# First channel product of a one-core attention and mixer kernel in seven block products, with pieces of the second between them

## The chip, the cores and the metric

The kernel runs on one core of one Trainium2 chip, in fp32 from end to end as the caller sees it. The metric is the device time of one execution in microseconds, the median of three runs. The engines are TensorE (PE, with its weight loads PEld), VectorE (DVE), ScalarE (ACT), GpSimd (POOL) and the DMA queue of SyncE (SP).

## The reference, cut to what matters

Three stages follow each other: a windowed attention, a mixer with a token and a channel part, and a gated channel block. The change lies in the channel part of the mixer (`_moe_ref`). The input `x` is the attention's output, 2 batches x 768 tokens x 512.

```python
def _moe_ref(x, w_tok1, w_tok2, w_ch1, w_ch2):
    xt = x.transpose(0, 2, 1)
    h = np.maximum(xt @ w_tok1, 0.0) @ w_tok2
    u = x + h.transpose(0, 2, 1)
    h2 = np.maximum(u @ w_ch1, 0.0) @ w_ch2      # 512 -> 1536 -> 512
    return u + h2

def _moe2_ref(x, mu_k, mu_r, w_k, w_v, w_r):
    ...
    k = np.maximum(xk @ w_k, 0.0)
    v = k * k @ w_v
    r = 1.0 / (1.0 + np.exp(-(xr @ w_r)))
    return r * v
```

## The kernel before

Every product runs on PE in fp32r. To keep precision each operand is split in a high half (rounded to fp32r) and a low half (the rest), and `three` (L944 to L948) issues high x high, high x low and low x high into the same PSUM bank. Making the halves is elementwise work: a copy that rounds (ACT, DVE or POOL) and a subtraction (DVE or POOL).

Tokens are cut in four groups g of 384 (`GR`), two to a batch; `u` holds, by 128 channels kk (`KT` = 4), the transposed activations. The order of work on each engine is written by hand, engine by engine, with semaphores between them; there is no scheduler. The stages that matter:

- Token stage (about 98 to 131 us): for 16 tiles, PE transposes x (L1017), multiplies the token part, DVE adds into `u` (L812). Beside it the weights of the channel part are split: DVE rounds (L794), POOL subtracts (L484). Between tiles 4 and 5 stand 36 matmuls of 512 columns of the token part's first product.
- Channel stage, L1034 to L1069: a loop over g. For each of 12 tiles f of 128 hidden channels, `first(f)` multiplies 4 kk x 3 matmuls of 384 columns into bank f % 2, ACT makes `rH` = ReLU (L614), DVE `rL` (L845), and `second(f - 1)` adds 4 x 3 matmuls of 384 columns into banks 2 to 5. All of W1 and half of W2 stand in SBUF with both halves before the stage begins; POOL makes the rest (L482, L484) early in it.
- Last stage, from about 332 us: a loop over g with `hidden(f)`, 12 matmuls of 384, and `value(f)`, 9 of 512, and the gate's 36 of 512. DVE has `k` (L871), `k2L` (L874), and the mixing of tokens (L833, L839).

Of the kernel before, what the change touches and what calls it, by code (L numbers as in the profile page):

```python
# [18 lines left out]
def build_program(nc, q, k, v, w_tok1, w_tok2, w_ch1, w_ch2, mu_k, mu_r, w_k, w_v, w_r, out):  # L19
# [28 lines left out]
    UG = GR + 1  # L48
    WIDE = 1024
    NWT, N1, N2, NK, NR, NV = 6, FC // 2, FC // 2, FK // 2, KT // 2, FK // 2  # L50

    ctx = ExitStack()
    with ctx:
# [32 lines left out]
        AS = 2 * N1 * W + 2 * 3 * W  # L86
        U0 = A0 + AS
        US = 4 * KT * NGR * UG
# [43 lines left out]

        reg = Region(A0, AS)
        W1H = reg.take("W1H", [P, N1, WIDE], F32R)
        W1L = reg.take("W1L", [P, N1, WIDE], F32R)
        W2aH = reg.take("W2aH", [P, 3, WIDE], F32R)
        W2aL = reg.take("W2aL", [P, 3, WIDE], F32R)
        reg = Region(X0, XS)
        W2bH = reg.take("W2bH", [P, 3, WIDE], F32R)
        W2bL = reg.take("W2bL", [P, 3, WIDE], F32R)  # L140
        WkH = reg.take("WkH", [P, NK, WIDE], F32R)
        WrH = reg.take("WrH", [P, NR, WIDE], F32R)
        reg = Region(T0, TS)
        uH = reg.take("uH", [P, KT, GR], F32R)
        uL = reg.take("uL", [P, KT, GR], F32R)
        WrL = Region(T0 + TS // 2, TS // 2).take("WrL", [P, NR, WIDE], F32R)
        WkL = Region(H0, HS).take("WkL", [P, NK, WIDE], F32R)

        reg = Region(A0, AS)
        xkH = reg.take("xkH", [P, KT, GR], F32R)  # L150
# [3 lines left out]
        assert reg.pos <= A0 + 5 * W  # L154
# [3 lines left out]
        k2 = [reg.take(f"k2{i}", [P, GR]) for i in range(2)]  # L158
        k2H = [reg.take(f"k2H{i}", [P, GR], F32R) for i in range(3)]
        k2L = [reg.take(f"k2L{i}", [P, GR], F32R) for i in range(3)]  # L160
        assert reg.pos <= A0 + 2 * N1 * W

        reg = Region(X0 + W, 2 * W)
        sg = [reg.take(f"sg{i}", [P, DM]) for i in range(RT)]
        u = at("u", [P, KT, NGR, UG], U0)
        reg = Region(H0, HS)
        h1H = reg.take("h1H", [P, B, TT, DM], F32R)
        h1L = reg.take("h1L", [P, B, TT, DM], F32R)
        reg = Region(R0, RS)
# [29 lines left out]
        wh_done, wp_done, wl_done = sem("wh_done"), sem("wp_done"), sem("wl_done")  # L199
# [81 lines left out]
        def w_dst(n):

            if n < PC2:
                return W1H[:, n - PC1, :], W1L[:, n - PC1, :]
            if n < PK:
                j = n - PC2
            elif n < PR:
                return WkH[:, n - PK, :], WkL[:, n - PK, :]
            elif n < PV:
                return WrH[:, n - PR, :], WrL[:, n - PR, :]  # L290
            else:
                j = n - PV
            return (W2aH[:, j, :], W2aL[:, j, :]) if j < 3 else (W2bH[:, j - 3, :], W2bL[:, j - 3, :])
# [3 lines left out]
        def _(sp):  # L297
# [62 lines left out]
            def load_piece(n, slot, src, by_rows, j, free=True):  # L360
                if free:
                    sp.wait_ge(wl_done, n - NSTG + 2)
                if by_rows:
                    dst, part = halves(stg[slot][:, :]), src[:, bass.ds(2 * j, 2), :]
                else:
                    dst, part = quarters(stg[slot][:, :]), src[:, :, bass.ds(256 * j, 256)]
                sp.dma_start(dst, part).then_inc(ld_w[slot], 16)

            sp.wait_ge(wl_done, NWT + 1)
            for slot in range(NSTG):  # L370
                load_piece(PC1 + slot, slot, w1_cols, False, slot, free=False)
            for slot in range(NSTG):
                load_piece(PC1 + NSTG + slot, slot, w1_cols, False, NSTG + slot)
            with sp.Fori(0, N2 // NSTG) as i:
                for slot in range(NSTG):
                    load_piece(PC2 + NSTG * i + slot, slot, w2_rows, True, NSTG * i + slot)
            for n in range(PK, PEND):
                first, src, by_rows = ((PK, wk_cols, False) if n < PR else (PR, wr_rows, True) if n < PV
                                       else (PV, wv_rows, True))
                load_piece(n, (n - PC1) % NSTG, src, by_rows, n - first)  # L380
# [10 lines left out]
        def _(pool):  # L391
# [96 lines left out]
        def _(act):  # L488
# [35 lines left out]
            for credited in (xl_done, av_done, wl_done, vs_summed, wr_done, o_done, x2_done, sg_done, mixl_done):  # L524
                act.sem_inc(credited, 1)
# [619 lines left out]
```

## Time and profile before

| what | us |
|---|---|
| runs, device time | 505.86, 504.46, 503.38; median 504.46 |
| span of the profiled execution | 501.4 |
| PE busy | 478.4 (95%) |
| DVE, ACT, POOL busy | 221.7, 191.6, 114.6 |
| channel stage, 131.4 to 331.9 | 200.5, of which PE busy 200.5 |

The profile is of one execution. Its own device time is not given beside its span; the median of the runs is 3.0 us above the span. Times within the trace count from the span's start. A matmul's end is modelled, so "busy" on PE does not say how fast it works; the distance between two starts does. A line number such as L948 is that of a helper where one issues many matmuls.

### The profile page before, as it was taken

Reading aid. Unit: us, or ns where it says so; the run is one execution under the profiler, and the core shown is the slowest. Engines: PE = TensorE matmul, PEld = TensorE weight load, DVE = VectorE, ACT = ScalarE, POOL = GpSimd, SP = SyncE. Lnnn points to the kernel's source line nnn. Section 1 sums busy time; section 2 is a strip of 40 time slices with the busy share of each in tenths; the row PEclk is TensorE's granted clock in tenths of the full one; section 3 lists DMA queues with packets and bytes.
Section 4 is the critical chain, followed back from the end, with each engine's and each line's share of the span. In section 5 each row is a group of like instructions: output and inputs, shape, how many; then the busy total and the mean of one; then the engine's idle time right before and its main releaser. Section 6 shows DMA issues by size and latency. Waiting matters only on the chain.

```text
span 501.4 us, 8399 instructions
## 1 busy us (share of the span) xinstructions
PE 478.4 (95%) x2968; PEld 444.9 (89%) x2968; DVE 221.7 (44%) x575; ACT 191.6 (38%) x424; POOL 114.6 (23%) x98
## 2 busy tenths in 40 slices
PE   4798789998999999999999999999999999999996
PEld 4677678787999999999999999999889989989985
DVE  5598887499411141114111411456436355444521
ACT  3799887424211121112111211345455256353411
POOL 6364553285999000000000024300000000000000
PEclk9999999999999999999999999999999999999999
DMA  9999997144443100000000010000010001001001
GB/s 196 181 208 215 228 213 186 46 126 129 166 149 145 43 1 0 0 0 0 0 0 0 0 42 0 0 1 0 1 49 14 0 21 42 0 0 63 0 0 63
DMA packets 48657, 31.70 MB, mean 63 GB/s; under 512 B 21248, under 2 KB 42496, under 8 KB 48640
## 3 DMA queue, kind: packets, MB, share of 16 engines
q1 hardware_dynamic: 48640, 31.49, 26.4%
q8 instruction: 9, 0.15, 0.1%
q14 instruction: 8, 0.07, 0.1%
HBM read 27.14 MB, written 3.15 MB: 60 GB/s over the span
## 4 chain that ended last, share of the span: by engine, by line
PE 84%; SPq 5%; DMA 5%; ACT 2%; issue 2%; DVE 1%; POOL 0%; ACTq 0%; POOLq 0%
PE bank L946 26%; PE bank L947 26%; PE bank L948 26%; DMA kn<-in_k_dram 4%; SPq L301 2%; PE bank L998 1%; SPq L310 1%; DMA v<-in_v_dram 1%; PE bank L976 1%; ACT e_sb L518 1%; PE bank L1017 1%; ACT qbd L498 1%; PE bank L895 1%; SPq L321 1%; PE bank L928 1%
## 5 line engine op out<-in xcount | busy, mean ns | idle before, releaser
L845 DVE SCALAR_TENSOR_TENSOR rL<-bank,rH 128x384 fp32r<-128x384 f32 x48 | 26.7, 557 | 148.2 <-ACT rH L614 148.2
L614 ACT ACTIVATE rH<-bank 128x384 fp32r<-128x384 f32 x48 | 23.6, 492 | 163.1 <-PE bank L948 158.7
L946 PE MATMUL bank<-uH,W1H 128*128 128x384 f32 x192 | 64.8, 337 | 0.0
L947 PE MATMUL bank<-uL,W1H 128*128 128x384 f32 x192 | 64.6, 336 | 0.0
L948 PE MATMUL bank<-uH,W1L 128*128 128x384 f32 x192 | 64.4, 336 | 0.0
L947 PE MATMUL bank<-xkL,WkH 128*128 128x384 f32 x128 | 43.3, 338 | 0.0
L946 PE MATMUL bank<-xkH,WkH 128*128 128x384 f32 x128 | 43.1, 337 | 0.0
L948 PE MATMUL bank<-xkH,WkL 128*128 128x384 f32 x128 | 42.8, 335 | 0.0
L947 PEld LDWEIGHTS bank<-uL,W1H 128*128 128x128 f32 x192 | 36.1, 188 | 0.0
L948 PEld LDWEIGHTS bank<-uH,W1L 128*128 128x128 f32 x192 | 36.0, 188 | 0.0
L946 PEld LDWEIGHTS bank<-uH,W1H 128*128 128x128 f32 x192 | 36.0, 188 | 0.0
L482 POOL CAST W2aH<-stg 128x1024 fp32r<-128x1024 f32 x3 | 3.1, 1040 | 142.3 <-PE bank L948 142.3
L871 DVE SCALAR_TENSOR_TENSOR k<-bank,kr 128x384 f32<-128x384 f32 x32 | 17.8, 556 | 38.7 <-ACT kr L631 38.6
L948 PE MATMUL bank<-rH,W2aL 128*128 128x384 f32 x96 | 32.3, 336 | 0.0
L948 PE MATMUL bank<-rH,W2bL 128*128 128x384 f32 x96 | 32.3, 336 | 0.0
L946 PE MATMUL bank<-rH,W2bH 128*128 128x384 f32 x96 | 32.2, 335 | 0.0
L947 PE MATMUL bank<-rL,W2bH 128*128 128x384 f32 x96 | 32.2, 335 | 0.0
L946 PE MATMUL bank<-rH,W2aH 128*128 128x384 f32 x96 | 32.2, 335 | 0.0
L947 PE MATMUL bank<-rL,W2aH 128*128 128x384 f32 x96 | 32.2, 335 | 0.0
L631 ACT ACTIVATE kr<-bank 128x384 f32<-128x384 f32 x32 | 15.7, 489 | 43.1 <-PE bank L948 42.7
L518 ACT ACTIVATE e_sb<-s_sb,nmx 128x120 f32<-128x120 f32 x96 | 29.7, 382 | 3.3 <-DVE nmx L693 3.3
L928 PE MATMUL bank<-kw,qbd 128*128 128x120 f32 x192 | 27.6, 292 | 1.8 <-ACT qbd L498 1.6
(131 smaller groups left out, 1093.2 us busy)
## 6 DMA issues: line engine op xcount, KB each, us to landing
stg<-in_moe_w_ch_dram SPq DMA_DIRECT2D x12, 512.0 KB, 3.6
vw<-in_v_dram SPq DMA_DIRECT2D x16, 240.0 KB, 4.9
kn<-in_k_dram SPq DMA_DIRECT2D x16, 192.0 KB, 3.8
qn<-in_q_dram SPq DMA_DIRECT2D x16, 192.0 KB, 4.4
v<-in_v_dram SPq DMA_DIRECT2D x16, 192.0 KB, 5.1
out_dram<-o_sb SPq DMA_DIRECT2D x12, 256.0 KB, 2.0
stg<-in_moe_w_k_dram SPq DMA_DIRECT2D x4, 512.0 KB, 3.5
stg<-in_moe_w_v_dram SPq DMA_DIRECT2D x4, 512.0 KB, 3.4
```

Of the source, the lines that this page charges most:

```text
L301: sp.dma_start(dst[par][:, h, :, :], src[bass.ds(2 * p + h, 1)].rearrange("o p t n -> (o p) t n")).then_inc(loaded[par], 16)
L310: sp.dma_start(dst, src[bass.ds(2 * p + h, 1)].rearrange("o p t n -> (o p) t n")).then_inc(ld_vw[par], 16)
L321: sp.dma_start(vw[par][LOC:COLS, :, :, :].rearrange("p t h n -> p t (h n)"), vsb[par][:, :, :].rearrange("p h n -> p (h n)").unsqueeze(1) ...
L518: act.activation(e_sb[par][:, n, :], s_sb[r][:, n, :], ACT.Exp, bias=nmx[:, r, n:n + 1], scale=-1.0).then_inc(exp_done, 1)
L614: act.activation(rH[f % 2][:, :], bank[f % 2][:, 0:GR], ACT.Relu).then_inc(rh_done, 1)
L631: act.activation(kr[f % 2][:, :], bank[f % 2][:, 0:GR], ACT.Relu).then_inc(kr_done, 1)
L845: dve.scalar_tensor_tensor(out=rL[f % 2][:, :], in0=bank[f % 2][:, 0:GR], scalar=0.0, in1=rH[f % 2][:, :].bitcast(F32), op0=ALU.max, op1=A ...
L871: dve.scalar_tensor_tensor(out=k2[f % 2][:, :], in0=bank[f % 2][:, 0:GR], scalar=0.0, in1=kr[f % 2][:, :], op0=ALU.max, op1=ALU.mult).then ...
L928: ins = pe.matmul(bS[gp][:, COLS * n:COLS * n + COLS], qbd[par][:, t, :], kw[par][:, t, :], start=True, stop=True)
L946: pe.matmul(dst, wH, mH, start=start, stop=False, **more)
L947: pe.matmul(dst, wH, mL, start=False, stop=False, **more)
L948: return pe.matmul(dst, wL, mH, start=False, stop=stop, **more)
```

## The change

The first channel product is computed by Strassen's scheme (in the form with shared sums) on 2 x 2 blocks. A block of W1 is 256 channels by 128 hidden channels, a block of u 256 channels by 384 tokens, so one run of the scheme (a "quad" q, 12 in all, 6 for each batch) makes two tiles of hidden channels for a whole batch of 768 tokens. Seven block products, each 2 x 3 matmuls of 384 columns, take the place of eight. `PRODUCTS` gives, for each, which sum of W1, which of u, the bank, and whether it opens or closes an accumulation.

- The seven combinations of W1 for a quad are made during the quad before: POOL does four sums of 256 columns (`sums_w1`), ACT rounds (`high_w1`), DVE subtracts (`low_w1`: 512, 256 and 1024 columns). W1 is read from HBM once for each batch, so there are 12 pieces in place of 6. The seven of u are made once for each batch: POOL `combine_u` (768 columns, 4 of them), ACT `high_u`, DVE `low_u`; batch 0's in the token stage, batch 1's in quads 0 to 5.
- Banks 0 and 1 hold sums that are shared, so products wait for DVE and ACT to have read a bank in the middle of a quad. DVE makes u2, u3, c22, c21 and c12 from a bank and an SBUF tile; ACT and DVE make the high and low half of R11 from the bank and of R22, R21, R12 from SBUF.
- The second product of quad q - 1 is cut in eight chunks, each 3 x (512 + 256) columns for one of two f and one of four d, which stand between the products of quad q as `GAPS` says; in the first quad of batch 1 as `GAPS_LAST` says.
- W2 is split anew for each batch by POOL (12 pieces); the weights of the last stage, which were split early in the channel stage, now come after it or between (`SLOT2`, `TAIL`): three in quads 6 to 8, seven behind the last product.
- DVE's residual adds are 512 and 2 x 256 columns wide and, for batch 0, stand in quad 6.

```diff
-            def channel(g):
-                def first(f):
...
-                    for kk in range(KT):
...
-                        ins = three(bank[f % 2][:, 0:GR], W1H[:, f // 2, c:c + P], W1L[:, f // 2, c:c + P],
-                                    uH[:, kk, :], uL[:, kk, :], kk == 0, kk == KT - 1)
...
+            def product(q, n):
+
+                b, slot = q // NFP, q % 2
+                w, m, bk, start, stop = PRODUCTS[n]
+                if n == 0:
+                    pe.wait_ge(w1_split, q + 1)
+                    if q:
+                        pe.wait_ge(sum_done, 5 * q)
+                if q % NFP == 0:
+                    pe.wait_ge(ul_done, NPROD * b + U_PLACE[m] + 1)
+                if n + 1 == P2:
+                    pe.wait_ge(p1_done, q + 1)
+                elif n + 1 == P7:
+                    pe.wait_ge(sum_done, 5 * q + 1)
+                elif n + 1 == P5:
+                    pe.wait_ge(rl_done, 4 * q + R11)
+                elif n + 1 == P4:
+                    pe.wait_ge(sum_done, 5 * q + 2)
+                elif n + 1 == P3:
+                    pe.wait_ge(sum_done, 5 * q + 3)
+                for kk in range(2):
+                    ins = three(bank[bk][:, 0:GR], w1H[slot][:, w, kk, :], w1L[slot][:, w, kk, :],
+                                ucH[b][:, m, kk, :], ucL[b][:, m, kk, :], start and kk == 0, stop and kk == 1,
+                                skip_group_check=True)
+                ins.then_inc(prod_done, 1)
...
+            GAPS, GAPS_LAST = (1, 1, 1, 1, 1, 1, 2), (2, 2, 2, 1, 1, 0, 0)
+            for q in range(NQ):
+                todo = list(CHUNKS) if q else []
+                for n in range(NPROD):
+                    product(q, n)
+                    for _ in range((GAPS_LAST if q == NFP else GAPS)[n] if q else 0):
+                        second(q - 1, *todo.pop(0))
+            for f, d in CHUNKS:
+                second(NQ - 1, f, d)
...
+            def quad(q):
...
+                plus(P6, u2, Bk, p1)
+                low_r(R11, 0, 0, A)
+                plus(P7, u3, Bk, p1)
+                if 1 <= q < NQ - 1:
+                    low_w1(q + 1, 0)
+                if q == NFP:
+                    residual(0, 0)
...
+                plus(P5, c22, A, u3)
+                low_r(R22, 1, 1, c22[:, :])
+                if q == NFP:
+                    residual(0, 1)
+                plus(P4, c21, Bk, p1)
+                if 1 <= q < NQ - 1:
+                    low_w1(q + 1, 1)
+                low_r(R21, 1, 0, c21[:, :])
+                for i in ahead:
+                    low_u(1, i)
+                if q == NFP:
+                    residual(0, 2)
+                plus(P3, c12, A, u2)
+                low_r(R12, 0, 1, c12[:, :])
+                if q == NFP:
+                    residual(0, 3)
```

The order of products is P1, P6, P2, P7, P5, P4, P3; P1, P2, P5 and P3 go to bank 0, P6, P7 and P4 to bank 1. The products' names and the sums' stand for their place in the scheme.

DVE in the channel stage before, two tiles of it (`rL` is the low half of the ReLU; the number behind a name tells buffers apart). This pattern fills a group:

```order
L845 SCALAR_TENSOR_TENSOR rL_130<-bank,rH_128 128x384
L844 REGISTER_ALU
L845 SCALAR_TENSOR_TENSOR rL_131<-bank,rH_129 128x384
L844 REGISTER_ALU
L845 SCALAR_TENSOR_TENSOR rL_130<-bank,rH_128 128x384
```

DVE now, from P6 to P3 of quad 2 (`u_111` is u2, `u_112` u3, `p_110` P1's copy, `c_113` c22, `c_101` c21, `c_105` c12, `ucL` the low half of batch 1's blocks):

```order
L1007 TENSOR_TENSOR u_111<-bank,p_110 128x384
L1012 SCALAR_TENSOR_TENSOR rL_108<-bank,rH_106 128x384
L1007 TENSOR_TENSOR u_112<-bank,p_110 128x384
L941 TENSOR_TENSOR w1L_97<-stg_56,w1H_93 128x512
L944 TENSOR_TENSOR w1L_97<-stg_56,w1H_93 128x256
L1007 TENSOR_TENSOR c_113<-bank,u_112 128x384
L1012 SCALAR_TENSOR_TENSOR rL_108<-c_113,rH_106 128x384
L1007 TENSOR_TENSOR c_101<-bank,p_110 128x384
L947 TENSOR_TENSOR w1L_97<-w1S_96,w1H_93 128x1024
L1012 SCALAR_TENSOR_TENSOR rL_108<-c_101,rH_106 128x384
L955 TENSOR_TENSOR ucL_104<-u,ucH_102 128x768
L1007 TENSOR_TENSOR c_105<-bank,u_111 128x384
```

One instruction of a tile has become a row of twelve (with the low half of R12 behind them thirteen), in which two inputs of most rows lie in SBUF.

POOL in the channel stage before (`stg` holds a weight as it came from HBM):

```order
L482 CAST W2bH<-stg_55 128x1024
L484 TENSOR_TENSOR W2bL<-stg_55,W2bH 128x1024
L482 CAST W2bH<-stg_56 128x1024
L484 TENSOR_TENSOR W2bL<-stg_56,W2bH 128x1024
L482 CAST W2bH<-stg_57 128x1024
L484 TENSOR_TENSOR W2bL<-stg_57,W2bH 128x1024
L482 CAST WkH<-stg_55 128x1024
L484 TENSOR_TENSOR WkL<-stg_55,WkH 128x1024
```

POOL now, from quad 2 on (`w1S` are sums of W1, `ucT` those of u, `w2` the piece of W2):

```order
L543 TENSOR_TENSOR w1S_96<-stg_56 128x256
L544 TENSOR_TENSOR w1S_96<-stg_56 128x256
L546 TENSOR_TENSOR w1S_96<-w1S_96,stg_56 128x256
L548 TENSOR_TENSOR w1S_96<-stg_56,w1S_96 128x256
L570 CAST w2H_117<-stg_57 128x1024
L572 TENSOR_TENSOR w2L_119<-stg_57,w2H_117 128x1024
L563 TENSOR_TENSOR ucT_103<-u,ucT_103 128x768
```

What was one run of splits at the stage's start is spread over all quads, with the sums ahead of each.

PE, a product of quad 1 and the piece behind it, where before 12 matmuls of `W1H` and 12 of `W2` followed each other:

```order
L1131 MATMUL bank<-ucH_98,w1H_93 128x384
L1132 MATMUL bank<-ucL_100,w1H_93 128x384
L1133 MATMUL bank<-ucH_98,w1L_97 128x384
L1264 MATMUL bank<-rH_106,w2H_117 128x512
L1265 MATMUL bank<-rH_106,w2H_117 128x256
L1264 MATMUL bank<-rL_108,w2H_117 128x512
L1265 MATMUL bank<-rL_108,w2H_117 128x256
L1264 MATMUL bank<-rH_106,w2L_119 128x512
L1265 MATMUL bank<-rH_106,w2L_119 128x256
```

Half of the second product's matmuls are now 512 columns wide, half 256, each pair with the same weights.

## Rows read from the trace of the kernel before

**Rows 1.** the page: the span and the chain that ended last:

```profile
span 501.4 us, 8399 instructions
...
PE 84%; SPq 5%; DMA 5%; ACT 2%; issue 2%; DVE 1%; POOL 0%; ACTq 0%; POOLq 0%
```

**Rows 2.** busy us (count) by stretch; then PE's clock, DMA share, GB/s:

```profile
98.00:131.40 33.40, 31.02 (x185) 28.38 (x181) 30.34 (x35) 10.62 (x22) 24.16 (x11) 1.00 0.41 127
131.40:331.90 200.50, 200.50 (x1154) 200.50 (x1153) 45.69 (x83) 33.56 (x69) 43.64 (x26) 1.00 0.09 29
331.90:373.30 41.40, 41.40 (x206) 37.08 (x205) 20.86 (x38) 18.32 (x35) 0.00 (x0) 1.00 0.02 9
```

**Rows 3.** PE in order of time: start, duration; 36 matmuls' first, and their follower:

```profile
103.63 0.39 PE L946 MATMUL bank<-xH,wt1H 128*128 128x512 f32 x1
...
111.83 0.49 PE L1017 MATMUL bank<-ident,u 128*128 128x128 f32 x3
```

**Rows 4.** weight loads: groups (busy us, mean ns), and eight by time:

```profile
L947 PEld LDWEIGHTS bank<-uL,W1H 128*128 128x128 f32 x192 | 36.1, 188 | 0.0
...
L928 PEld LDWEIGHTS bank<-kw,qbd 128*128 128x128 f32 x192 | 25.6, 208 | 2.4 <-issue 2.0 <-DVE nmx L693 0.4
...
27.20 0.97 PEld L928 LDWEIGHTS bank<-kw,qbd 128*128 128x128 f32 x8
```

**Rows 5.** groups of DVE and ACT by shape: busy us, mean ns:

```profile
L845 DVE SCALAR_TENSOR_TENSOR rL<-bank,rH 128x384 fp32r<-128x384 f32 x48 | 26.7, 557 | 148.2 <-ACT rH L614 148.2
...
L839 DVE TENSOR_TENSOR xkL<-mix_x,xkH 128x384 fp32r<-128x384 f32 x16 | 8.9, 555 | 0.6
...
L884 DVE TENSOR_TENSOR o_sb<-bank,sg 128x512 f32<-128x512 f32 x12 | 8.3, 692 | 29.5 <-ACT sg L644 29.5
...
L614 ACT ACTIVATE rH<-bank 128x384 fp32r<-128x384 f32 x48 | 23.6, 492 | 163.1 <-PE bank L948 158.7 <-DVE u L864 4.4
...
L582 ACT ACTIVATE uH<-u 128x384 fp32r<-128x384 f32 x4 | 2.1, 519 | 0.0
...
L570 ACT ACTIVATE xH<-u 128x128 fp32r<-128x128 f32 x2 | 0.6, 300 | 0.0
```

**Rows 6.** groups of POOL by shape; weight transfers (KB, us to landing):

```profile
L484 POOL TENSOR_TENSOR W2aL<-stg,W2aH 128x1024 fp32r<-128x1024 f32 x6 | 14.4, 2394 | 4.5 <-DVE W2aH L794 4.2
...
L457 POOL TENSOR_TENSOR xL<-u,xH x6 | 10.1, 1688 | 4.1 <-DVE xH L724 4.1
...
L438 POOL TENSOR_TENSOR v<-v 96x256 f32<-96x256 f32 x8 | 5.8, 726 | 0.6
...
L482 POOL CAST W2aH<-stg 128x1024 fp32r<-128x1024 f32 x3 | 3.1, 1040 | 142.3 <-PE bank L948 142.3
...
stg<-in_moe_w_ch_dram SPq DMA_DIRECT2D x12, 512.0 KB, 3.6
```

**Rows 7.** POOL and DVE in order of time, where they meet:

```profile
117.05 2.38 POOL L484 TENSOR_TENSOR W1L<-stg,W1H 128x1024 fp32r<-128x1024 f32 x1 [1.10 <-DVE W1H L794]
...
117.36 2.49 DVE L804 TENSOR_TENSOR uL<-u,uH 128x384 fp32r<-128x384 f32 x1
...
120.23 0.54 DVE L804 TENSOR_TENSOR uL<-u,uH 128x384 fp32r<-128x384 f32 x1
...
135.34 2.41 POOL L484 TENSOR_TENSOR W2bL<-stg,W2bH 128x1024 fp32r<-128x1024 f32 x1
...
136.30 0.56 DVE L845 SCALAR_TENSOR_TENSOR rL<-bank,rH 128x384 fp32r<-128x384 f32 x1 [1.52 <-ACT rH L614]
```

**Rows 8.** PE's two waits in the token stage, in order of time:

```profile
120.36 0.45 PE L946 MATMUL bank<-wt2H,h1H 128*128 128x384 f32 x1 [1.15 <-DVE u L812]
...
124.77 0.45 PE L946 MATMUL bank<-wt2H,h1H 128*128 128x384 f32 x1 [1.23 <-DVE u L812]
```

**Rows 9.** PE early in the span, in order of time:

```profile
9.45 3.74 PE L928 MATMUL bank<-kw,qbd 128*128 128x120 f32 x16 [1.65 <-ACT qbd L498]
...
23.80 1.05 PE L928 MATMUL bank<-kw,qbd 128*128 128x120 f32 x8
```

More of the change, by code:

```diff
@@ L85, in build_program @@
         A0 = C0 + CS
[L86 removed]
+        AS = 2 * NFP * W + 2 * 3 * W
         U0 = A0 + AS
[L88 removed]
+        US = 4 * KT * B * SQ
         H0 = U0 + US
@@ L149, in build_program @@
-        reg = Region(A0, AS)
+        rH = [reg.take(f"rH{i}", [P, 2, S], F32R) for i in range(2)]
+        rL = [reg.take(f"rL{i}", [P, 2, S], F32R) for i in range(2)]
+        reg = Region(R0, RS)
+        p1, u2, u3, c22 = [reg.take(name, [P, GR]) for name in ("p1", "u2", "u3", "c22")]
+        u = at("u", [P, KT, B, SQ], U0)
+        reg = Region(H0, HS)
+        h1H = reg.take("h1H", [P, B, TT, DM], F32R)
+        h1L = reg.take("h1L", [P, B, TT, DM], F32R)
+        reg = Region(H0, HS)
+        w2H = [reg.take(f"w2H{i}", [P, WIDE], F32R) for i in range(2)]
@@ L150, in build_program @@
+        w2L = [reg.take(f"w2L{i}", [P, WIDE], F32R) for i in range(2)]
+        WkH, WkL, WvH, WvL = [None] * NK, [None] * NK, [None] * NV, [None] * NV
+        reg = Region(UC0, A0 + AS - UC0)
+        for j in range(2):
+            WkH[j] = reg.take(f"WkH{j}", [P, WIDE], F32R)
+            WkL[j] = reg.take(f"WkL{j}", [P, WIDE], F32R)
         xkH = reg.take("xkH", [P, KT, GR], F32R)
@@ new lines, in build_program @@
+        R11, R22, R21, R12 = range(1, 5)
+        U_AHEAD = ((0,), (1,), (2,), (3,), (4, 6), (5,))
+        T_AHEAD = ((3,), (4,), (6,), (5,))
+        XR_AFTER = {1: (0, 1), 2: (2,), 3: (3,), 4: (4,)}
+        MIXED_AFTER = {NQ - 3: (0, 1), NQ - 2: (2, 3), NQ - 1: (4,)}
+        SLOT2 = [("w2", n) for n in range(NFP + 1)]
+        SLOT2 += [("wk", 0), ("w2", NFP + 1), ("wk", 1), ("w2", NFP + 2), ("wv", 0)]
+        SLOT2 += [("w2", n) for n in range(NFP + 3, NQ)]
+        TAIL = [("wk", 2), ("wv", 1), ("wk", 3), ("wv", 2), ("wv", 3), ("wr", 0), ("wr", 1)]
@@ L369, in _ @@
             sp.wait_ge(wl_done, NWT + 1)
[L370 to L380, printed above, removed]
+            load_w1(0)
@@ L487, in _ @@
+            pool.wait_ge(prod_done, NPROD * NQ)
+            for kind, n in TAIL:
+                if (kind, n) == ("wv", 1):
+                    pool.wait_ge(rl_done, 4 * NQ)
+                split(kind, n)
         @block.scalar
@@ L868, in last @@
+            for q in range(NQ):
+                quad(q)
+            for d in range(KT):
+                residual(1, d)
+            dve.wait_ge(x2_done, 6 * B)
             def last(g, more):
```

499 lines of the change are left out of this document (307 added, 192 removed).

## The prediction, made before the changed kernel was run

> **What bounds the kernel now.** The page comes first: the span is 501.4 us and the chain that ended last is 84% TensorE (PE) [rows 1]. Next the table by stage [rows 2]. In the stage that the change rewrites, 131.4 to 331.9 us, PE is busy for all of 200.5 us, its clock column reads 1.00 (2.4 GHz), and VectorE (DVE) and ScalarE (ACT) work 45.7 and 33.6 us of it. So PE's own stream sets this stage, and the gain must come from fewer columns on PE. Third, how far apart two matmuls start when PE never waits: for 384 columns 200.5 us over the stage's 1152 (the table's 1154 has two of its neighbours), 0.174 us, and for 512 columns 0.2278 us, 36 of them from 103.63 to 111.83 [rows 3]. The two differ by 128 columns at 2.4 GHz, so a matmul costs its columns plus about 33 cycles.
>
> **Matmuls removed.** Before, the first product issues 4 groups x 12 tiles x 4 x 3 = 576 matmuls of 384 columns. After, 12 quads x 7 products x 2 x 3 = 504. That is 72 fewer: 72 x 0.174 = **-12.5 us**.
>
> **Second product, recut.** 576 matmuls of 384 columns become 288 of 512 and 288 of 256, the same columns. By columns plus 33 cycles a 256 costs 0.120 us, and the pair 0.348 us against 2 x 0.174: **0**. No row has 256 columns of this type. The floor is the weight load, which every matmul repeats, also where the line before used the same weights [rows 4]; eight loads in a row took 0.97 us at 0.21 us each, so one can follow another after 0.11 us, just under 0.120. The dear end is that a 256 costs like a 384: 288 x 0.053 = +15 us. I take 0, since both known sizes lie on the line and the load fits.
>
> **The chain inside a quad.** Before, DVE had one step per tile of 4.17 us, 0.557 us long. Now each quad has five sums and four low halves on DVE, four high halves and a copy on ACT, plus the splits of the next W1 piece and, for six quads, of batch 1's blocks. The unit on PE is 1.04 us, for a product (6 x 0.174) and for a piece of the second product (3 x 0.348). Durations [rows 5]: sum or low half of 384, 0.56, from PSUM or SBUF; high half, 0.49 from PSUM and 0.52 from SBUF. For other sizes I use the slopes: DVE 0.555 to 0.69 for 384 to 512 gives 0.42, 0.96 and 1.22 for 256, 768 and 1024; ACT 0.30 to 0.52 for 128 to 384 gives 0.84 for 768. Back to back on one engine each takes about 0.09 less.
>
> *Quad 0 has no pieces between its products.* P5 waits for R11: P2's end, ACT 0.49, DVE 0.56 is 0.3 us more than the one product beside it. After P5 (ends 5.68 us after the quad's start) DVE does c22 (6.29), waits for ACT, low R22 (7.46), c21 (7.93), ACT again, low R21 (9.10), a block of batch 1, 0.96 plus a POOL collision (10.4), and c12 (11.0). Quad 1's first product waits for c12, and PE was done at 7.7. **+3.6 us** (3.4 to 4.0).
>
> *Quads 1 to 5 and 7 to 11.* From P4's end to the next quad's first product lie a piece, P3 and two pieces, 4.17 us. In them DVE does c21, low W1 (1024), low R21, a block (768), c12: 0.47 + 1.13 + 0.47 + 0.87 + 0.56 = 3.5, and with about 0.3 us for the end of the matmul and the semaphores, 3.8. The margin is 0.4 us. Where two blocks stand (q = 4) it is -0.5. So **+1.0 us** if GpSimd (POOL) gets in the way only there, see below.
>
> *Quad 6* closes batch 0's second product early (GAPS_LAST), so nothing stands after P4 or P3, and DVE also has six residual adds (0.69 each). From c22 on: low R22, two residuals, c21, low W1 1.22, low R21, a residual, c12, in all 1.2 + 1.2 + 0.5 + 1.1 + 0.5 + 0.6 + 0.5 = 5.6, with about 0.9 for two POOL sums in the way 6.4 us from P3's start, of which P3 covers 1.04: **+5.3 us** (3.2 if POOL never interferes). Before P3 0.2 more.
>
> **POOL and DVE on SBUF.** What decides here is in [rows 7]. A DVE subtraction with both inputs in SBUF (uL) takes 0.54 us alone and 2.49 us when it starts 0.3 us after a POOL instruction that ends at 119.43; it ends 0.42 us after that. One that reads PSUM and SBUF (rL) takes 0.56 inside POOL's 2.41. So a collision makes the later one wait for the earlier one's end. Seven DVE instructions of a quad are of the first kind, and POOL issues in the same quad four sums of 256 columns (0.73 each), a cast (1.04) and a subtraction (2.39) of a w2 piece, and in some quads a block (1.69) or another weight [rows 6]. POOL's sums start when the quad's last product has ended, just as DVE does its tail: one collision costs up to 0.7 us against a margin of 0.4. The Trainium skill, page "SBUF — State Buffer", section "Who interferes with whom", says that a DVE instruction with two SBUF inputs and a GpSimd one that reads SBUF exclude each other for a whole instruction and that issue order decides; these rows agree (2.49 against 0.54). Without this rule the time would be that of rival A.
>
> **Other moves.** Each stall also slows the first matmul after it by about 0.1 us [rows 8]: +0.3 in all. In the token stage (98.0 to 131.4) DVE is busy 30.3 of 33.4 us and POOL 24.2 [rows 2], DVE's share swollen by its waits for POOL. POOL's nine W1 and W2a subtractions of 2.39 us go, and DVE's casts with them; in come 8 sums and 4 blocks on POOL (8 x 0.73 + 4 x 1.69 = 12.6 us) and 7 blocks and two W1 pieces on DVE (7 x 0.96 + 2 x 2.33 = 11.4 us). PE waited 1.15 and 1.23 us for DVE there [rows 8]; I keep about half of it, so **-1.2 us**. The w1 loads are issued when the piece before is split, land 3.6 us later [rows 6] and have most of a quad; the w2 loads likewise: 0.
>
> **In the last stage** POOL now splits seven weights back to back, 7 x 3.4 = 24 us from the end of the last product, which is 8 us before the last stage. Before it was idle there [rows 2]. DVE's k2L, mix and xr subtractions all read SBUF twice and wait up to 2.4 us each. A tile with its value product lasts 4.1 us on PE. Tiles 1 and 2 have four or five such instructions, so the ReLU step of tile 2 comes late: **+2.0 us** (0 to 4).
>
> **Sum.** -12.5 + 3.6 + 1.0 + 5.5 + 0.3 - 1.2 + 2.0 = **-1.3 us**. The span would be 500.1. The median of the runs, 504.46, lies 3.0 us above the span, and nothing outside the span changes: 504.46 - 1.3 = **503.2 us**. A measurement of this kernel can tell 0.5%, 2.5 us, from no change.
>
> **Rivals.**
> *A. POOL and DVE miss each other.* For it: POOL is idle half of a quad. Against it: its sums start with DVE's tail. Then the sum is -12.5 + 3.4 (quad 0) + 0.4 (quads 1 to 5) + 3.2 (quad 6) + 0.3 - 2.1 (token stage) + 0 (last stage) = -7.3, **497.2**. Chance 0.22.
> *B. Slower: POOL is first each time.* If POOL's first sum is issued a tenth of a us before DVE's block, and DVE waits for all of an instruction's recorded time, the sum is -12.5 + 4.0 (quad 0) + 4.2 (quads 1 to 5: 0.5 each, 2.2 for q = 4) + 6.4 (quad 6) + 1.9 (quad 8, POOL's Wv split across low R22) + 0.5 - 0.3 (token stage) + 4.1 (last stage) = +8.3, **512.8**; half of it, 507 to 509, is as likely. It decides from a tail 0.4 us longer than mine. Chance 0.20, with 507 or more.
> *C. The clock.* PE now stands still for 3.3 and 5.3 us at a time; in the stage before the change it never did. A low rate is seen near the start [rows 9]: 16 matmuls in 3.74 us at 9.45, 8 in 1.05 at 23.80, 0.234 against 0.131 each, near 1.2 against 2.4 GHz, with the clock column at 1.00, which seems to have no record there. If each gap is followed by a stretch of its own length at half speed, that loses 1.7 and 2.7 us: +4, **507**. Chance 0.12. The Trainium skill, page "TensorE: Matmul & The Clock Gate", section "What you observe" and those after it, tells of two levels, 1.2 and 2.4 GHz, the lower one following idleness; of these gaps no run here shows it yet.
> *D. The 256-column matmuls cost like 384.* **518**. Chance 0.05.
> The forecast and its near surroundings have 0.41.
>
> **From these the numbers.** Faster by over 0.5% (below 501.9): A and 0.11 of the forecast's 0.41, together 0.33. Within: 0.28 of the forecast and half of C, 0.34. Slower: B, D, the other half of C and 0.02 of the forecast, 0.33. The range leaves out D and the far half of B, and the edge beyond A: 496.0 to 510.5.
>
> **What would show it.** In the changed profile: 1080 matmuls in the rewritten stage at 0.174 on average, and a 256 after 0.12; PE's idle before quad 1 near 3.3 and before quad 7 near 5.3, released by DVE's c12; DVE's two-SBUF instructions of over 1.5 us exactly where POOL runs; the first product of quads 2 to 6 with gaps of 0 to 0.5; a gap near 2 us in the last stage's tile 4, released by DVE's ReLU step. It is wrong if the gap before quad 7 is under 3 or over 7, if PE waits for DMA or POOL's split, or if PE's clock falls.

## The result, and the profile after

The changed kernel took 510.01 us (median of 4 runs, 508.96 to 510.25), the kernel before 503.92 in the same comparison (4 runs, 502.51 to 505.86): a ratio of 1.013, 95% interval 1.010 to 1.015. The change made the kernel slower by 6.1 us. The forecast was 503.2, with 496.0 to 510.5 as its range; 510.0 lies inside the range, just under its upper end.

The page of the changed kernel, its profiled execution (508.96 us), against [rows 1]. In the clock row each digit is one fortieth of the span:

```profile
span 507.1 us, 8294 instructions
...
PEclk9999899999989999999799999998999999999999
...
PE 80%; DVE 6%; DMA 4%; issue 3%; ACT 3%; POOL 2%; SPq 2%; DVEq 0%; ACTq 0%; POOLq 0%
```

DVE is now 6% of the chain that ended last, where it was 1%, and the clock row has digits below 9 in the slices with 143, 242 and 348 us (and with 55, in the attention, which the change leaves alone). The same stages as in [rows 2], columns as there (the clock is the third from the right), and three short windows in which the clock falls:

```profile
98.00:130.30 32.30, 31.33 (x196) 29.03 (x197) 24.72 (x36) 18.49 (x34) 15.79 (x13) 1.00 0.05 17
130.30:333.10 202.80, 192.97 (x1082) 178.92 (x1081) 112.25 (x165) 58.57 (x106) 107.23 (x80) 0.97 0.22 72
333.10:374.60 41.50, 39.49 (x190) 35.38 (x189) 26.59 (x36) 17.48 (x34) 16.05 (x9) 0.96 0.09 31
...
142.00:146.00 4.00, 3.80 (x15) 3.54 (x16) 0.98 (x2) 1.02 (x2) 3.92 (x4) 0.67 0.00 0
...
246.00:250.00 4.00, 4.00 (x16) 3.67 (x16) 2.53 (x4) 0.49 (x1) 0.77 (x1) 0.61 0.40 131
...
346.00:352.00 6.00, 4.15 (x14) 4.13 (x15) 4.82 (x7) 2.43 (x6) 3.39 (x2) 0.72 0.00 0
```

The rewritten stage lasts 202.8 us where it lasted 200.5, with 72 matmuls fewer. PE is idle for 9.8 us of it. Most of the rest is in the clock column, which read 1.00 in all three stages before: in the three short windows it is 0.6 or 0.7. TensorE in order of time, its waits and what comes behind them:

```profile
142.20 0.41 PE L1131 MATMUL bank<-ucH,w1H 128*128 128x384 f32 x1 [3.92 <-DVE c L1007]
...
207.52 0.41 PE L1131 MATMUL bank<-ucH,w1H 128*128 128x384 f32 x1 [0.93 <-DVE c L1007]
...
243.96 0.66 PE L1131 MATMUL bank<-ucH,w1H 128*128 128x384 f32 x1 [4.78 <-DVE c L1007]
244.42 0.52 PE L1132 MATMUL bank<-ucL,w1H 128*128 128x384 f32 x1
244.74 0.52 PE L1133 MATMUL bank<-ucH,w1L 128*128 128x384 f32 x1
...
249.55 0.39 PE L1264 MATMUL bank<-rH,w2H 128*128 128x512 f32 x1
249.78 0.28 PE L1265 MATMUL bank<-rH,w2H 128*128 128x256 f32 x1
249.90 0.39 PE L1264 MATMUL bank<-rL,w2H 128*128 128x512 f32 x1
...
347.85 0.41 PE L1131 MATMUL bank<-xkH,WkH 128*128 128x384 f32 x1 [2.01 <-DVE k L1056]
```

Behind the wait of 4.78 us two matmuls of 384 columns start 0.32 us apart (244.42, 244.74), not 0.174: 1.2 GHz. From 249.2 on the spacing is normal again, with a 256 every 0.12 us as forecast. The same holds from 143.3 to 146.8 and from 348.4 to 351.6. Against the normal spacing (0.174, 0.231, 0.12 us) these stretches lose 1.55, 2.45 and 1.56 us.

Where the 5.7 us of span went: the rewritten stage starts 1.1 us earlier (130.35 for 131.42), lasts 2.3 longer, and the last stage lasts 4.5 longer (173.9 for 169.5). The earlier start is two things. The token stage, from the first transpose of x to the first channel matmul, is 1.8 us shorter (31.5 for 33.4), and the attention ahead of it was 0.8 us longer in this execution (98.8 for 98.1). The attention differs from one execution to the next, whatever the kernel: in the twelve profiles it ends between 96.9 and 101.6 us, while the token stage lasts 33.4 us in all six of the kernel before and its pauses, and 31.5 in the other six.

### The profile page after: what moved, and what is told of

It reads as the page before. It is cut to its first block, busy times and chain, and to the rows that moved or that the text cites. A ratio compares the mean times of both kernels' runs of the same rounds, so it can differ in the third digit from the quotient of the medians.

```text
span 507.1 us, 8294 instructions
## 1 busy us (share of the span) xinstructions
PE 472.7 (93%) x2896; PEld 425.3 (84%) x2896; DVE 288.6 (57%) x654; ACT 223.3 (44%) x470; POOL 184.9 (36%) x163
## 4 chain that ended last, share of the span: by engine, by line
PE 80%; DVE 6%; DMA 4%; issue 3%; ACT 3%; POOL 2%; SPq 2%; DVEq 0%; ACTq 0%; POOLq 0%
PE bank L1131 18%; PE bank L1132 18%; PE bank L1133 18%; PE bank L1264 13%; PE bank L1265 6%; DMA kn<-in_k_dram 3%; DMA v<-in_v_dram 2%; PE bank L1183 2%; PE bank L1161 1%; SPq L357 1%; PE bank L1113 1%; PE bank L1080 1%; PE bank L1202 1%; ACT e_sb L634 1%; DVE rL L1012 1%
## 5 line engine op out<-in xcount | busy, mean ns | idle before, releaser
L1131 PE MATMUL bank<-ucH,w1H 128*128 128x384 f32 x168 | 58.1, 346 | 9.8 <-DVE c L1007 9.6
L1132 PE MATMUL bank<-ucL,w1H 128*128 128x384 f32 x168 | 57.2, 341 | 0.0
L1133 PE MATMUL bank<-ucH,w1L 128*128 128x384 f32 x168 | 57.2, 340 | 0.0
L1264 PE MATMUL bank<-rL,w2H 128*128 128x512 f32 x96 | 38.1, 397 | 0.0
L1264 PE MATMUL bank<-rH,w2L 128*128 128x512 f32 x96 | 38.1, 397 | 0.0
L1264 PE MATMUL bank<-rH,w2H 128*128 128x512 f32 x96 | 38.1, 397 | 0.0
L1133 PE MATMUL bank<-WvH,k2L 128*128 128x512 f32 x96 | 37.8, 394 | 0.0
L1132 PE MATMUL bank<-WvL,k2H 128*128 128x512 f32 x96 | 37.8, 393 | 0.0
L1131 PE MATMUL bank<-WvH,k2H 128*128 128x512 f32 x96 | 37.3, 389 | 0.0
L1132 PEld LDWEIGHTS bank<-ucL,w1H 128*128 128x128 f32 x168 | 32.7, 195 | 0.0
```

The costliest lines, as they stand in the source:

```text
L1131: pe.matmul(dst, wH, mH, start=start, stop=False, **more)
L1132: pe.matmul(dst, wH, mL, start=False, stop=False, **more)
L1133: return pe.matmul(dst, wL, mH, start=False, stop=stop, **more)
L1264: pe.matmul(wide, w, r[slot][:, f, 0:512], start=begin, stop=end, skip_group_check=True)
```

## The experiments

All are compared with the kernel before on the same chip. Where two experiments are set against each other, the stages of their profiles say more than the totals, since the attention differs as told above. A "slow stretch" is a row of matmuls of 384 columns 0.32 us apart.

**Is it the clock, or the neighbours?** `e1_fill` keeps PE busy in the three waits:

```diff
+                if q == 1:
+                    keep_busy(21, bank[2][:, 0:GR], w1H[0][:, 6, 1, :], ucH[0][:, 2, 1, :])
+                if q == NFP + 1:
+                    pe.wait_ge(x2_done, 1)
+                    keep_busy(25, bank[2][:, 0:GR], w1H[0][:, 6, 1, :], ucH[1][:, 2, 1, :])
...
+                    if f == 4 and isinstance(g, int):
+                        keep_busy(10, bank[7][:, 0:GR], WkH[0][:, 0:P], xkH[:, 0, :])
...
-            with pe.Fori(0, NGR) as g:
+            last(0)
+            with pe.Fori(1, NGR) as g:
```

The last lines take the first group of the last stage out of its loop, so that only this one gets matmuls to fill with.

> The changed kernel with TensorE kept busy in its three long waits: 21 matmuls of 384 columns before quad 1 and 25 before quad 7 into an accumulator that nothing reads any more, 10 before tile 4 of the first last-stage group; each group starts its own sums afresh, so nothing of the result changes. The three gaps of 3.92, 4.78 and 2.01 us stay as long as they are, since DVE ends them, but TensorE is idle for less than 0.7 us in each. Theory 'clock' (the stretches with matmuls of 384 columns 0.32 us apart, 3.2, 5.0 and 3.2 us long, follow TensorE's own standstill): all three stretches vanish, the granted clock reads 1.00 from 126 to 370 us, and the time falls by 1.55 + 2.45 + 1.56 = 5.5 us, to about 504.5. Rival 'neighbours' (TensorE is slowed by what DVE, POOL and the DMAs do in SBUF just then): the stretches stay where they are, and the time stays at 510.

Measured: 504.20 us (10 runs), ratio 1.000 (0.998 to 1.003). The waits behind the filling are 0.48 us before quad 7, 0.22 before tile 4 and none before quad 1. The first two lines are TensorE in order of time, the others windows as above:

```profile
235.35 4.50 PE L1276 MATMUL bank<-ucH,w1H 128*128 128x384 f32 x25
240.33 0.41 PE L1131 MATMUL bank<-ucH,w1H 128*128 128x384 f32 x1 [0.48 <-DVE c L1007]
```

```profile
142.00:146.00 4.00, 4.00 (x25) 3.75 (x24) 0.79 (x2) 0.75 (x2) 3.92 (x2) 1.00 0.09 20
...
242.00:246.00 4.00, 4.00 (x25) 3.76 (x24) 1.09 (x2) 0.32 (x2) 1.60 (x1) 1.00 0.31 86
...
346.00:352.00 6.00, 6.00 (x31) 5.40 (x31) 4.17 (x9) 3.66 (x8) 0.00 (x0) 1.00 0.02 4
```

DVE and POOL do the same work, and DVE still ends the waits before quad 7 and tile 4, yet the clock reads 1.00 and no slow stretch is left. So the stretches follow TensorE's own standstill, and "neighbours" falls. The granted clock over the whole execution is 0.978 to 0.988 in the four runs of the changed kernel and 0.990 to 1.000 in these ten. The medians, 510.0 and 504.2, lie 5.8 us apart. In the profiles the rewritten and the last stage together last 372.1 us for 376.8, 4.7 less, where the stretches had lost 5.6; of the 0.9 us between, 0.7 are three new waits of about 0.25 us before other quads, and such waits come and go without an edit (see `e2_xr_later` below `e7_pool_waits`). The rest of the difference lies in the attention. What is left is the change without the clock's loss: no gain to be seen (ratio 1.000, with an interval that holds the sum's -1.3 us too).

**Where the last stage's wait comes from.** `e2_xr_later`:

```diff
-        XR_AFTER = {1: (0, 1), 2: (2,), 3: (3,), 4: (4,)}
+        XR_AFTER = {3: (0, 1), 4: (2,), 5: (3,), 6: (4,)}
```

> The changed kernel with the steps that prepare the gate's input two tiles later in every group of the last stage (tiles 3 to 6 in place of 1 to 4). Theory: the wait of 2.01 us before tile 4 comes from these steps, which read SBUF twice and stand behind POOL's late splits, ahead of the ReLU step of tile 2. It goes (0 to 0.3 us left), and with it the slow stretch behind it, 1.56 us: -3.5 us, about 506.5. Rival 1 (the ReLU step is late because of k2L alone, which also waits for POOL): 1 to 2 us of wait stay and the time is 508 to 510. Rival 2 (the steps are late for the gate instead): a new wait before the gate of 1 us or more in each of four groups, 508 or more.

Measured: 506.40 us (10 runs), ratio 1.003 (1.000 to 1.006); the last stage lasts 170.1 us for 173.9, and PE has no wait in it. DVE in order of time, of the changed kernel and then of this one:

```profile
339.20 2.74 DVE L1059 TENSOR_TENSOR k2L<-k,k2H 128x384 fp32r<-128x384 f32 x1 [0.59 <-ACT k2H L780]
341.86 4.07 DVE L983 SCALAR_TENSOR_TENSOR mix_x<-u,mu,mix_t 128x384 f32<-128x384 f32 x2
345.85 1.39 DVE L988 TENSOR_TENSOR xrL<-mix_x,xrH 128x384 fp32r<-128x384 f32 x1
347.16 0.55 DVE L1056 SCALAR_TENSOR_TENSOR k<-bank,kr 128x384 f32<-128x384 f32 x1
```

```profile
343.31 0.55 DVE L1056 SCALAR_TENSOR_TENSOR k<-bank,kr 128x384 f32<-128x384 f32 x1
344.44 2.73 DVE L1059 TENSOR_TENSOR k2L<-k,k2H 128x384 fp32r<-128x384 f32 x1 [0.59 <-ACT k2H L780]
347.10 0.55 DVE L1056 SCALAR_TENSOR_TENSOR k<-bank,kr 128x384 f32<-128x384 f32 x1
```

This k2L lasts 2.7 us in both (0.56 before the change): POOL's splits still stand in its way. But a tile is 4.2 us long, and k2L alone fits. Only with the gate's steps (4.07 and 1.39 us) in the same tile does the ReLU step `k` come late.

**DVE's work, or its order?** `e3_sums_first` issues the same instructions in another order:

```diff
                 plus(P5, c22, A, u3)
-                low_r(R22, 1, 1, c22[:, :])
-                if q == NFP:
-                    residual(0, 1)
+                if 1 <= q < NQ - 1:
+                    low_w1(q + 1, 1)
                 plus(P4, c21, Bk, p1)
-                if 1 <= q < NQ - 1:
-                    low_w1(q + 1, 1)
+                low_r(R22, 1, 1, c22[:, :])
+                plus(P3, c12, A, u2)
                 low_r(R21, 1, 0, c21[:, :])
-                for i in ahead:
-                    low_u(1, i)
-                if q == NFP:
-                    residual(0, 2)
-                plus(P3, c12, A, u2)
+                if q == NFP:
+                    residual(0, 1)
                 low_r(R12, 0, 1, c12[:, :])
+                for i in ahead:
+                    low_u(1, i)
                 if q == NFP:
+                    residual(0, 2)
                     residual(0, 3)
```

> The changed kernel with another order in DVE's queue for a quad: the low W1 part right after c22, the sums c21 and c12 ahead of the low halves of R22 and R21, and the blocks of batch 1 and the residual adds behind the last low half; the same instructions. Theory (what TensorE waits for is DVE's queue order, not DVE's amount of work): c12 ends 0.6 us after the last product, so 0.7 us of wait before quad 1 (was 3.92), none in quads 1 to 5 (was 0.93), 0.7 before quad 7 and 0.9 before its first piece for a residual add (was 4.78); no standstill over 1 us, so no slow stretches in this stage (4.0 us). In all -3.2 - 0.9 - 3.2 - 4.0 = -11.3, about 498.7 us. Rival (DVE and POOL have too much to do in the quads, whatever the order): waits of 1 to 3 us reappear before products or pieces of quads 2 to 6, and less than half is won, 504 or more.

Measured: 498.48 us (4 runs), ratio 0.988 (0.984 to 0.991). TensorE's waits of 0.5 us and more in the stage, and the window over the stage:

```profile
138.56 0.41 PE L1130 MATMUL bank<-ucH,w1H 128*128 128x384 f32 x1 [0.74 <-DVE c L1007]
...
234.39 0.41 PE L1130 MATMUL bank<-ucH,w1H 128*128 128x384 f32 x1 [1.23 <-DVE c L1007]
```

```profile
129.80:321.70 191.90, 189.06 (x1082) 175.35 (x1081) 118.22 (x165) 58.46 (x106) 109.48 (x80) 1.00 0.23 76
```

The stage falls from 202.8 to 191.9 us though DVE is busier in it (118.2 us for 112.3). Of these 10.9 us, some 7.0 are idle time of PE (2.8 for 9.8) and 4.0 the two slow stretches, of which none is left. The waits were a matter of order. The last stage's wait is still there (2.22 us, and a stretch behind it that loses 1.56).

**POOL in DVE's way.** `e7_pool_waits` moves one wait on POOL:

```diff
-                    pool.wait_ge(prod_done, NPROD * (n - 1))
+                    pool.wait_ge(sum_done, 5 * (n - 1))
```

> The changed kernel with one wait of POOL moved: its sums for the next W1 piece begin when DVE has made c12, not when the quad's last product has ended. So POOL is out of DVE's way in the tail of a quad. Theory (each DVE instruction with two SBUF inputs that meets POOL's sums lasts longer by what is left of the POOL instruction): low R21 of quad 0 falls from 1.13 to 0.56 us and the block from 1.47 to 0.96, so the wait before quad 1 falls from 3.92 to about 2.9 us; low R21 of quad 6 from 1.07 to 0.56, the wait before quad 7 from 4.78 to about 4.2; before quad 5 from 0.93 to 0.5. The slow stretches stay. In all -2 us, about 508. Rival (the exclusion plays no part, DVE's instructions are long for another reason): waits unchanged, 510. If POOL's later start makes the next W1 piece late, TensorE waits for DVE before a quad's first product in every quad, 512 or more.

Measured: 506.07 us (10 runs), ratio 1.005 (1.002 to 1.008). DVE before quad 1, in the changed kernel and then here:

```profile
139.06 1.13 DVE L1012 SCALAR_TENSOR_TENSOR rL<-c,rH 128x384 fp32r<-128x384 f32 x1 [0.59 <-ACT rH L748]
140.11 1.47 DVE L955 TENSOR_TENSOR ucL<-u,ucH 128x768 fp32r<-128x768 f32 x1
```

```profile
140.07 0.56 DVE L1012 SCALAR_TENSOR_TENSOR rL<-c,rH 128x384 fp32r<-128x384 f32 x1 [0.59 <-ACT rH L748]
140.80 0.96 DVE L955 TENSOR_TENSOR ucL<-u,ucH 128x768 fp32r<-128x768 f32 x1 [0.18 <-ACT ucH L710]
```

Both fall to their lone times, and the waits become 3.05 and 4.20 us (3.92 and 4.78) and 0.38 before quad 5 (0.93), 2.0 us less in all, as expected. But new waits of 0.79 and 0.55 us appear before other quads, so PE's waits in the stage fall by 0.7 us only. So the exclusion is real, and this edit moves more of its cost than it saves. The time fell further than the 508 expected because two slow stretches are missing in this profile: none behind the 3.05 us before quad 1, none behind the 2.01 us in tile 4. That was not foreseen, and it led to the runs below.

How little decides such a collision is seen in `e2_xr_later`, whose edit lies in the last stage. Its wait before quad 1 was 3.33 us, not 3.92. DVE's low R21 and POOL's second sum, in the changed kernel and then there:

```profile
139.06 1.13 DVE L1012 SCALAR_TENSOR_TENSOR rL<-c,rH 128x384 fp32r<-128x384 f32 x1 [0.59 <-ACT rH L748]
...
139.05 0.73 POOL L544 TENSOR_TENSOR w1S<-stg 128x256 f32<-128x256 f32 x1
```

```profile
139.13 0.56 DVE L1012 SCALAR_TENSOR_TENSOR rL<-c,rH 128x384 fp32r<-128x384 f32 x1 [0.59 <-ACT rH L748]
...
139.14 1.13 POOL L544 TENSOR_TENSOR w1S<-stg 128x256 f32<-128x256 f32 x1
```

In the first POOL starts 0.01 us ahead and DVE takes twice its time; in the second DVE is 0.01 us ahead and POOL is the one that takes longer. That run also has a new wait of 0.57 us before a later quad. So waits of half a microsecond come and go without an edit that reaches them.

**How long must PE stand still?** Here POOL's memsets hold TensorE in the kernel before, in groups 1 and 2. The first try:

```diff
+                    if (g, f) in PAUSES:
+                        pe.sem_inc(pause_go, 1)
+                        pe.wait_ge(pause_end, list(PAUSES).index((g, f)) + 1)
```

> The kernel before, with its channel loop written out and TensorE made to stand still eight times in groups 1 and 2, every third tile (12.5 us apart), for about 0.95, 1.2, 1.55, 1.8, 2.05, 2.5, 2.9 and 3.8 us, each ended by memsets on POOL, which is otherwise idle there, and DVE at a fifth of its time; nothing else changes. Theory 'clock': no slow matmuls behind the pauses up to about 1.2 us (0.93 and 1.23 had none), a slow stretch behind those of 2.05 us and more (2.01, 3.92 and 4.78 had one) of 3 to 5 us, each costing 1.5 to 2.5 us; which of the two holds for 1.55 and 1.8 us is open. With 16.8 us of pauses and four such stretches the time is some 504 + 17 + 7 = 528 us. Rival 'neighbours': no matmul is slow behind any pause, and the time is 521 us.

Measured: 507.8 us (one run), and one wait only, of 0.64 us where 3.8 was meant; this run tells nothing of the clock. The next four let the last matmul signal, and differ in the lengths and the order of the eight pauses:

```diff
-                        second(f - 1)
+                        ins = second(f - 1)
+                        if (g, f + 1) in PAUSES:
+                            ins.then_inc(pause_go, 1)
```

> The run before (e4_pauses) made hardly a pause: its signal to POOL was an instruction of its own in TensorE's queue and fired 3 us or more before the matmuls ahead of it had ended. Here the signal hangs on the last matmul before each pause, at tiles 2, 5, 8 and 11 of groups 1 and 2 of the kernel before. POOL's memsets took 0.69, 0.93, 1.34, 1.59, 1.84, 2.34, 2.76 and 3.74 us; with 0.3 us for the two signals TensorE stands still for about 1.0, 1.2, 1.65, 1.9, 2.15, 2.65, 3.05 and 4.05 us, in this order, 17.7 us in all. Theory 'clock': full rate behind the first two, a slow stretch of 3 to 5 us behind each from 2.15 on, 1.5 to 2.5 us of loss each; open for 1.65 and 1.9. Time 504 + 17.7 + 8 = about 530 us. Rival 'neighbours' (SBUF traffic of DVE and POOL slows the matmuls): no slow stretch, 522 us.

> The same with the eight pauses in another order: about 4.05, 1.0, 3.05, 1.2, 2.65, 1.65, 2.15 and 1.9 us. If the length of a pause alone decides, the same pauses have a slow stretch as in the run with rising lengths, and each stretch has the same loss whatever its place; if what went before or chance of time decides, pauses near 2 us change sides between the two runs and equal pauses lose differently by 0.5 us or more (two pauses before quad 1, 3.92 and 3.33 us long in two runs, lost 1.55 and 2.75 us, which speaks for this).

> The kernel before with eight equal pauses of about 1.95 us at tiles 2, 5, 8 and 11 of groups 1 and 2. So far a standstill of 1.95 to 2.01 us was followed by a slow stretch in two of four cases (2.01 in the changed kernel and 1.95 in the mixed run; not 2.01 in the run where POOL waits, nor 1.95 in the rising run). If length alone decides, all eight do the same; if also when it falls, some have a slow stretch and some not. 504 + 15.6 us of pauses + 1.5 for each slow stretch: 520 with none, 532 with eight, about 526 if it is half of them.

> The same with eight pauses of about 3.05 us. A wait of 3.05 us before quad 1 had no slow stretch behind it in the run where POOL waits, while pauses of 2.44 and 2.86 had one in both runs. If length decides, all eight have one, 504 + 24.4 + 8 x 1.6 to 2.7 = 541 to 550 us; if that wait of 3.05 was no exception, one or more of the eight has none.

Measured, one run each: 527.8, 528.8, 529.0 and 541.3 us. The pauses of the first two came out at 0.80, 1.05, 1.45, 1.70, 1.95, 2.44, 2.86 and 3.85 us. That of 1.95 us has no slow stretch behind it in `e5_pauses_up` and one in `e6_pauses_mixed`; that of 3.85 us has one in both, with a loss of 1.6 and 2.7 us. So length alone does not decide. Two of the eight equal pauses of `e10_pauses_305`, and the windows behind two pauses of 1.95 us in `e9_pauses_195`:

```profile
191.08 0.45 PE L956 MATMUL bank<-uH,W1H 128*128 128x384 f32 x1 [3.03 <-POOL scratch L478]
191.37 0.34 PE L957 MATMUL bank<-uL,W1H 128*128 128x384 f32 x1
191.54 0.34 PE L958 MATMUL bank<-uH,W1L 128*128 128x384 f32 x1
...
206.90 0.60 PE L956 MATMUL bank<-uH,W1H 128*128 128x384 f32 x1 [3.03 <-POOL scratch L478]
207.30 0.53 PE L957 MATMUL bank<-uL,W1H 128*128 128x384 f32 x1
207.62 0.53 PE L958 MATMUL bank<-uH,W1L 128*128 128x384 f32 x1
```

```profile
222.50:226.50 4.00, 3.93 (x22) 3.93 (x23) 0.56 (x1) 0.49 (x1) 0.02 (x1) 1.00 0.00 0
237.30:241.30 4.00, 3.98 (x14) 3.98 (x15) 0.00 (x0) 0.17 (x1) 0.00 (x0) 0.57 0.00 0
```

Equal pauses in equal surroundings, and one has a slow stretch and the other none (in the windows the clock is 1.00 and 0.57). All standstills of over 0.7 us after 130 us, from the profiles of the changed kernel and of all experiments but the filled one:

| TensorE stood still | with a slow stretch behind it | loss of each |
|---|---|---|
| 0.74 to 1.70 us | none of 15 | 0 |
| 1.95 to 2.01 | 7 of 12 | 1.55 to 1.67 |
| 2.22 to 2.86 | 5 of 5 | 1.54 to 1.56 |
| 3.03 to 3.33 | 8 of 10 | 1.42 to 2.93 |
| 3.85 to 4.78 | 6 of 6 | 1.55 to 2.72 |

Losses are against the normal spacing. The first matmul behind a gap is 0.08 to 0.1 us late even at full clock; this is left out where that matmul is not slow itself, and is in the loss where it is. Length decides between never and nearly always; the loss hardly depends on it (3.33 us cost 2.75 and 3.92 us 1.55; 18 of the 26 lie between 1.5 and 1.7). Near 2 us, and now and then at 3, it differs from one standstill to the next; what else decides was not found. DVE is nearly idle in the pauses, so the neighbours have no part here either. The Trainium skill, page "TensorE: Matmul & The Clock Gate", section "What's actually happening", says that idleness brings the low level back, and that the number of slow matmuls at a kernel's start differs from run to run. The traces agree with the first. What they show of the second is in the kernel's middle: the wait of 2.01 us in tile 4 has a slow stretch behind it in the changed kernel and none in `e7_pool_waits`.

**A version meant to beat both.** `e8_combined` is `e3_sums_first` and `e2_xr_later` together with

```diff
-            GAPS, GAPS_LAST = (1, 1, 1, 1, 1, 1, 2), (2, 2, 2, 1, 1, 0, 0)
+            GAPS, GAPS_LAST, GAPS_NEXT = (1, 1, 1, 1, 1, 1, 2), (2, 2, 1, 1, 1, 1, 0), (0, 2, 1, 1, 1, 1, 2)
```

where `GAPS_NEXT` holds for quad 7.

> A version meant to beat both: the order of e3_sums_first (sums ahead of low halves), the gate's steps two tiles later (e2_xr_later), batch 0's last pieces spread so that one stands between P4 and P3 of quad 6, and P6 of quad 7 ahead of that quad's first piece, which waits for a residual add. Theory: e3_sums_first measured 498.5; the wait of 2.22 us in tile 4 and the slow stretch behind it (1.46) go as they went in e2_xr_later, and of the 1.88 us of waits around quad 7 about 0.6 stay: 498.5 - 3.7 - 1.3 = 493.5 us, granted clock 1.00 throughout, no wait of TensorE over 1 us after 100 us. Rival (another wait of 2 us or more comes up once these are gone): 496 or more.

Measured: 491.90 us (5 runs, 491.06 to 493.33), ratio to before 0.977 (0.974 to 0.980).

```profile
span 490.1 us, 8295 instructions
...
PEclk9999999999999999999999999999999999999999
...
PE 84%; DMA 5%; SPq 3%; ACT 2%; issue 2%; DVE 2%; POOL 1%; ACTq 0%; DVEq 0%; POOLq 0%
```

The chain is 84% TensorE again, as in [rows 1]. One wait over 1 us is left, 1.24 us before quad 7 (expected: none). The stage lasts 191.0 us, 9.6 less than before the change: the 12.5 us of removed matmuls, less 2.2 of waits and 0.7 of the rest. The token stage is 1.9 us shorter than before the change and the last stage 0.7 longer, so 10.8 of the 11.3 us of span come from the kernel's edits, and the rest from an attention that ended earlier.

## Why the prediction was wrong, point by point

- **Matmuls removed, -12.5, and the recut, 0.** Right. A 256 starts its successor 0.12 us later, so rival D (518) falls. A 512 in these pairs takes 0.23, as in [rows 3].
- **Quad 0, +3.6.** 0.21 and 3.92 us, 4.1 in all. POOL was in the way twice (1.13 for 0.56, 1.47 for 0.96), not once.
- **Quads 1 to 5, +1.0.** 0.93, at the place named.
- **Quad 6, +5.5.** 4.78 us before quad 7 and nothing before P3. The forecast's 3.2 "if POOL never interferes" does not come out of its own steps, 5.6 less the 1.04 that P3 covers, which give 4.6; with POOL's collision gone `e7_pool_waits` has 4.20. So rival A was a microsecond or more too low.
- **Restarts, +0.3.** They and matmuls a few ns slower came to 0.9 in the stage.
- **Token stage, -1.2.** It is 1.8 us shorter, with one wait of 0.81 us where [rows 8] had two: nearer to rival A's 2.1. The attention ahead of it was 0.8 us longer in this execution, which no term could foresee.
- **Last stage, +2.0.** The wait is 2.01 us, in tile 4, behind DVE's ReLU step, as forecast; `e2_xr_later` shows that the place and the reason were right, while the exact hit, out of "0 to 4", was luck. Another 0.9 us has no term in the sum. Of it 0.7 is spread over the stage: a tile with its value product lasts 4.19 us for 4.15 in all four groups, also in `e2_xr_later` and `e8_combined`, where the stage has no wait and no slow stretch and is still 0.7 us longer than before the change. What makes it so was not tried.
- **The clock, 0.** This is the step that failed. The other terms as measured add up to -12.5 + 4.1 + 0.9 + 4.8 + 0.9 - 1.8 + 2.0 + 0.9 = -0.7, where the prediction had -1.3; single terms were off by up to 0.9 us and partly cancel. The three slow stretches, at nothing in the forecast's sum, add 1.55 + 2.45 + 1.56 = 5.6. With the 0.8 us of the attention that is the 5.7 us of span. The prediction named "if PE's clock falls" as a sign that it is wrong, and the clock fell. That 510.0 still lies inside the range is owed to rival B, for which the range was drawn that wide, and B's course of events did not come about.

Rival C had the mechanism, and by luck nearly the price of the first two stretches (1.7 + 2.7 forecast, 4.0 measured; in `e2_xr_later` they lost 5.2 behind waits that were no longer), but 0.12 of the chance, as if it were another course of events. It was not: its condition, TensorE at rest for 3.3 and 5.3 us, stood in the forecast's own sum. The two had to be added. It also left out the third standstill, which the sum priced at 2.0 us, and its rule (a stretch as long as the gap) was wrong in kind: `e10_pauses_305` has 1.42 and 2.93 us of loss behind equal pauses. With 1.5 to 2.5 us behind each of three standstills, a price that only these runs gave, the forecast would have been 508 to 511.

Rivals A and B turned on POOL and DVE. The waits came out between the two, near the forecast's middle way; `e7_pool_waits` takes 2.0 us off three of them and puts 1.3 on others. The forecast's 3.0 us "above the span" was read from two different things, the median of the runs and the span of one execution. Wherever a run's time and its own span are both on record they lie 1.7 to 2.1 us apart, before and after the change alike. So nothing outside the span changed, and the profile of the kernel before was, by this, of an execution some 1 us quicker than the median.

## What to carry to other kernels

Where a change puts a standstill of TensorE of 2 us or more on the path, between matmuls as dense as here, add the clock's share, mostly 1.5 to 2.5 us for each, to the sum itself; it is no rival to it. Before calling such a change a loss, look at the order in the queue of the engine that ends the wait: here sums ahead of low halves, the gate's steps two tiles later and the pieces around quad 7 spread otherwise turned 1.3% slower into 2.3% faster, with the same work. If the wait can't be moved, matmuls into an accumulator that nobody reads keep the clock up; three such fillings saved 5.6 us here, and the two stages got shorter by 4.7.

## What the runs showed that was not expected

- A standstill of 1.95 us can be enough for 1.2 GHz, and one of 3.05 us can pass without it (table above). The slow matmuls begin with the first one behind the gap or up to 1.5 us later.
- A semaphore increment that is an instruction of its own in TensorE's queue fires while matmuls ahead of it still run. In `e4_pauses` the memsets of the longest pause start at 267.76 us, 3.2 us before the last matmul ahead of the wait ends, and leave only 0.64 us of wait. Hung on that matmul (`e5_pauses_up`) they start 0.1 us behind its end, and the wait is 3.85 us.
- POOL suffers from DVE as well: a sum of 256 columns for the W1 pieces took 1.07 us on average over 12 (0.72 to 1.50), against 0.73 for one of that size in [rows 6]. In `e7_pool_waits`, where they wait for DVE's sums, all 12 take 0.73 to 0.75.
